# An attention block with two dense layers: the second layer's first pair split earlier, and its turns moved behind the next block product

## The reference

```python
def _moe_ref(x, w_in, w_out, s, b):              # first dense layer, d_ff 2048
    r = np.maximum(x @ w_in, 0.0)
    return (s * (r * r) + b) @ w_out

def _moe2_ref(x, w_in, w_out, g_ln):             # second dense layer, d_ff 1024
    h = x @ w_in
    e = np.exp(h - h.max(-1, keepdims=True))
    solu = h * (e / (e.sum(-1, keepdims=True) + 1e-09))
    mu, var = solu.mean(-1), ((solu - mu) ** 2).mean(-1)
    return ((solu - mu) / np.sqrt(var + 1e-06) * g_ln) @ w_out
```

## Time and profile before

| | |
|---|---|
| median of 3 runs | 860.84 us (860.62 to 861.01) |
| profiled execution | 860.25 us |
| its span in the trace | 858.0 us |
| PE busy | 843.0 us, 98% |
| DVE busy | 514.4 us, 60% |
| ACT busy | 339.7 us, 40% |
| POOL busy | 341.3 us, 40% |

### The profile page before, as it was taken

The page is one execution under the profiler, slowest core; times in us unless marked ns, Lnnn a source line. Parts: engine busy times, 40 slices in busy tenths (PEclk is TensorE's granted clock), DMA queues, the critical chain, the costliest instruction groups (busy, mean ns, idle before and its releaser), DMA issues.

```text
span 858.0 us, 13135 instructions
## 1 busy us (share of the span) xinstructions
PE 843.0 (98%) x4912; PEld 745.5 (87%) x4912; DVE 514.4 (60%) x1052; ACT 339.7 (40%) x607; POOL 341.3 (40%) x452
## 2 busy tenths in 40 slices
PE   8999999999999999999999999999999999999998
PEld 7899999999888888888888889999997878888886
DVE  7766657666547865433443344335767987777763
ACT  6665555556442223222322232224345433333322
POOL 5665656565659993000000000001548753334400
PEclk9999999999999999999999999999999999999999
DMA  8665666665403332000000000000101100000001
GB/s 147 147 144 130 152 140 140 145 132 126 118 14 98 111 99 74 1 0 1 1 1 0 1 1 1 1 1 1 50 26 50 36 26 25 26 24 13 25 25 49
DMA packets 86365, 49.35 MB, mean 58 GB/s; under 512 B 65056, under 2 KB 73248, under 8 KB 86304
## 3 DMA queue, kind: packets, MB, share of 16 engines
q1 hardware_dynamic: 83760, 47.94, 23.2%
q10 hardware_dynamic: 2544, 0.59, 0.4%
HBM read 27.28 MB, written 4.72 MB: 37 GB/s over the span
## 4 chain that ended last, share of the span: by engine, by line
PE 85%; DVE 10%; issue 3%; ACT 1%; POOL 1%; ACTq 0%; POOLq 0%; DVEq 0%
PE ps_h L1256 7%; PE ps_h L1257 7%; PE ps_h L1258 7%; PE ps_y L1271 7%; PE ps_y L1272 7%; PE ps_y L1273 7%; PE ps_v L650 7%; PE ps_s L565 4%; PE ps_r L1721 3%; PE ps_r L1720 3%; PE ps_r L1719 3%; PE ps_hid L1654 3%; PE ps_hid L1656 3%; PE ps_hid L1655 3%; DVE spent L967 3%
## 5 line engine op out<-in xcount | busy, mean ns | idle before, releaser
L1373 DVE TENSOR_TENSOR xT<-xT 128x512 f32<-128x512 f32 (+1 forms) x80 | 61.7, 772 | 125.6 <-ACT xT L1331 125.5
L1273 PE MATMUL ps_y<-g_hi,wout 128*128 128x512 f32 (+1 forms) x320 | 117.5, 367 | 0.0
L1272 PE MATMUL ps_y<-g_lo,wout 128*128 128x512 f32 (+1 forms) x320 | 117.5, 367 | 0.0
L1271 PE MATMUL ps_y<-g_hi,wout 128*128 128x512 f32 (+1 forms) x320 | 117.4, 367 | 0.0
L1557 POOL TENSOR_TENSOR win<-stage,win 128x512 fp32r<-128x512 f32 x2 | 2.6, 1296 | 281.8 <-ACT win L1788 281.8
L650 PE MATMUL ps_v<-v_raw,pT 128*128 128x65 f32 (+1 forms) x960 | 107.6, 254 | 1.2 <-DVE t_loc L1065 1.2
L650 PEld LDWEIGHTS ps_v<-v_raw,pT 128*128 128x128 f32 (+1 forms) x960 | 101.3, 173 | 6.9 <-issue 4.7
L967 DVE CUSTOM_DVE_ANT_0 spent<-ps_s,mask 128x576 f32<-128x576 f32 (+4 forms) x160 | 81.6, 540 | 42.4 <-PE ps_s L565 41.8
L1256 PE MATMUL ps_h<-x_hi,win 128*128 128x512 f32 (+1 forms) x280 | 103.0, 368 | 0.0
L1258 PE MATMUL ps_h<-x_hi,win 128*128 128x512 f32 (+1 forms) x280 | 102.8, 367 | 0.0
L1257 PE MATMUL ps_h<-x_lo,win 128*128 128x512 f32 (+1 forms) x280 | 102.8, 367 | 0.0
(11 more groups left out here) (211 smaller groups left out, 1805.1 us busy)
## 6 DMA issues: line engine op xcount, KB each, us to landing
stacked<-cut SPq DMA_DIRECT2D x56, 288.0 KB, 5.1
out<-res SPq DMA_DIRECT2D x18, 256.0 KB, 2.0
v_raw<-in_v SPq DMA_DIRECT2D x32, 128.0 KB, 3.2
stage<-in_moe_w_in SPq DMA_DIRECT2D x16, 256.0 KB, 2.7
stage<-in_moe_w_out SPq DMA_DIRECT2D x16, 256.0 KB, 2.6
k_raw<-in_k SPq DMA_DIRECT2D x28, 128.0 KB, 2.6
q_raw<-in_q SPq DMA_DIRECT2D x28, 128.0 KB, 3.6
stage<-in_moe_w_in SPq DMA_DIRECT2D x4, 512.0 KB, 3.5
```

Source lines behind the costliest of these rows:

```text
L1271: pe.matmul(out, wout[:, f, HI, w], g_hi[:, r, 0:n], start=(f == 0), stop=False)
L1272: pe.matmul(out, wout[:, f, HI, w], g_lo[:, r, 0:n], start=False, stop=False)
L1273: ins = pe.matmul(out, wout[:, f, LO, w], g_hi[:, r, 0:n], start=False, stop=(f == FT - 1))
L1373: dve.tensor_tensor(r, r, r, ALU.mult).then_inc(square_done, 1)
```

## The change

Three things are changed.

1. `round_y(0)` moves from the aside at f = 14 to the one at f = 12 on ScalarE, and `cut_lows(dve, 0)` from f = 14 to f = 13 on VectorE, ahead of low_crossed(1, BOTTOM). The rounding of pair 0 waits for output 9 of the last chunk in place of output 11; the cut of its low part now waits for output 10 and the cut of the sums' low part for output 11.
2. In the pairs p = 2 to 8 TensorE's `turn(a)` comes after `sums_product(p)`, and `turn(b)` after `shared_product(p)`.
3. In the same pairs VectorE does `join_first(p)` before both halves of `turned_low(a)`, and `join_shared(p)` before both halves of `turned_low(b)`.

No instruction of computation is added or removed.

```diff
     def y_is_free(eng, p):
         if p == 0:
-            freed.second_weights(eng, 11)
+            freed.second_weights(eng, 9)
...
         def cut_sums(p):
             y = y_of[p % 2]
+            if p == 0:
+                freed.second_weights(pool, 11)
             pool.wait_ge(s_hi_done, p + 1)
...
     def cut_lows(eng, p):
 
         y, a, b = y_of[p % 2], 2 * p, 2 * p + 1
+        if p == 0:
+            freed.second_weights(eng, 10)
         eng.wait_ge(y_hi_done, RAW * p + 1)
...
             upper_tile(p)
+            sums_product(p)
             turn(a)
-            sums_product(p)
             lower_products(p)
+            shared_product(p)
             turn(b)
-            shared_product(p)
             upper_ends(p)
...
             if f == 12:
                 high_crossed(1, TOP)
+                round_y(0)
             if f == 13:
                 round_sums(0)
                 high_crossed(1, BOTTOM)
-            if f == 14:
-                round_y(0)
...
             if f == 13:
+                cut_lows(dve, 0)
                 low_crossed(1, BOTTOM)
-            if f == 14:
-                cut_lows(dve, 0)
...
                 a, b = 2 * p - 2, 2 * p - 1
+                join_first(p)
                 turned_low(a, 0)
                 turned_low(a, 1)
-                join_first(p)
                 join_second(p)
+                join_shared(p)
                 turned_low(b, 0)
-                join_shared(p)
                 turned_low(b, 1)
```

## The result

| | before | after |
|---|---|---|
| median of 5 runs each | 861.01 us (860.62 to 861.76) | 856.79 us (856.63 to 857.42) |
| ratio | | 0.995, 95% interval 0.9936 to 0.9965 |
| profiled execution | 860.25 us | 856.63 us |
| its span | 858.0 us | 854.5 us |

The two traces differ by 3.5 us of span. In the later sessions 14 of 55 executions of the kernel before took 861.5 to 862.0 us, with a mean granted clock of 0.997 or 0.998, and the others 859.8 to 861.1 us, with 0.999 or 1.0, while none of the 77 executions of kernels with the earlier split showed less than 0.999; what ties the two together is not shown.

A forecast was written before the change was run, and what follows sets the result against it. TensorE, busy 98% of the span, was taken as the bound, so only its waits could be won: 1.6 + 1.36 = 2.9 us off 860.25 gives 857.3, plus 0.59 a median of 857.9 us; range 857.2 to 859.6.

The forecast's parts named there:

- Gap 1: TensorE's wait between output(4, 13) and upper_tile(0), 2.40 us with its slow first product; forecast to close wholly.
- What is queued behind: Load and pair 1's sums behind L1911 come 0.55 us later; exponentials(0) start at 658.15, only 0.7 earlier.
- The chain up to turn(2): VectorE from the exponentials on: join_second(1) and normalise(2) 1.55 us earlier, normalise(2) ending at 686.05.
- gap 2: TensorE's wait before turn(2) for a normalised tile, 1.08 us; 0.55 forecast to be left.
- the full 3.48: Both TensorE gaps closed, 2.40 + 1.08 us: the most the change can bring.
- Part 2: turn(a) behind sums_product(p): 1.36 us less TensorE work before turn(2); the six later pairs cost nothing.
- Rival D: Slower: turn(b) waits for tile a's low part behind join_first(p), one product each in seven pairs, 867.4 us; chance 0.04.
- From the span to the median: The median taken 0.59 us above the profiled execution, turning 857.3 into 857.9 us.
- B: Low cuts caught twice, GpSimd's scaling going ahead of L1911: gain 2.2 us, time 858.7; chance 0.22.
- C: The gap only changes place and only the turns' move pays: 1.08 to 1.36 us, time 859.5 to 859.8; chance 0.14.
- E: No effect: TensorE's waits come from something later than VectorE's low part, time stays 860.8 us; chance 0.02.

The follow-up runs named there:

- the split alone: Kernel before with only the earlier split and finer waits, TensorE's and VectorE's loops as before: 858.21 against 860.32 us, ratio 0.9972.
- the run with the sums first: Changed kernel with ScalarE rounding the sums at f = 12 and the rows at f = 13: 857.95 us against 860.60 for the kernel before.

## Why the prediction was wrong

The size was wrong, the direction and the places were right. Two terms of the sum were mis-sized. The first is the 1.6 us by which VectorE would be ahead at turn(2): it was 2.13. The second is the 0.59 us from the profiled execution to the median, which was 0.16 for the changed kernel. The paths of both follow.

**Gap 1** closed wholly, as forecast: pair 0 starts at 646.73 for 646.81 forecast. The split's placing was right; its gain in time alone is 2.1 us, which the run of the split shows.

**What is queued behind.** This step failed. I let the second cut be caught behind cut_sums; it was not, since VectorE's two cuts followed each other without a gap and GpSimd waited (2.68 for 2.40). I added 0.55 to the load and the sums; L1914 did end 0.34 later, at 646.09, but GpSimd went on only 0.19 later and made that up in its sums, whose first had met VectorE before and now did not (1.04 before, 0.73 after). That the first sum was longer because of VectorE is read off the overlap of the rows and was not tested. So exponentials(0) started at 657.56, not at 658.15.

**The chain up to turn(2).** "Only 0.7 earlier ... This is the step that limits the gain" was mis-sized. From the exponentials on I moved VectorE by 0.66 (for the 0.70 of the step before); spread_of(0) came 1.63 earlier (661.98 for 663.61): 1.3 of it from the exponentials themselves, and the rest because ScalarE's two exponentials now follow each other at once (VectorE's maxima are long done) and the multiplications and copies behind them take 3.20 (658.78 to 661.98) where they took 3.52 (660.09 to 663.61 in the trace of before). join_second(1) then came just as TensorE's product was ready, and moved by the full 2.42; the run with the weights behind the exponentials shows that this product is its limit. From there 0.3 were lost again, which I had not reckoned with: normalise(0) (L1973 at 665.62) now runs beside GpSimd's scaling (L1601, 664.88 to 666.25) and took 1.18, where it took 0.81 at 668.05 before, with the scaling over at 667.69. So VectorE was 2.13 earlier at turn(2); that the scaling is the cause is read off the overlap. The 0.55 us that I left of gap 2 were 0.06. That is 0.5 us of the error: the full 3.48, which I had as the upper bound, is what happened. That it came out so exactly is luck: the 2.13 and the 1.36 of sums_product(2) make 3.49, with nothing to spare. The two operations that meet, VectorE's and GpSimd's in the kernel after:

```profile
665.62 1.18 DVE L1973 TENSOR_SCALAR expo<-expo,small 128x1024 f32<-128x1024 f32 x1
```

```profile
664.88 1.37 POOL L1601 TENSOR_SCALAR stage<-stage,ln_gain 128x512 f32<-128x512 f32 x2
```

**Part 2** was right: 1.36 of work against a wait of 1.37 with the split alone, nothing in the later pairs, and the slack in both orders as computed there. Rival D's mechanism, a turn(b) that waits for tile a behind join_first, is real but needs one half of the change without the other: the run with TensorE's old order gives its price, 0.4 us a pair.

**From the span to the median.** I took the median of before, 860.84, 0.59 above its profiled execution, and kept this distance for the kernel after. There it was 0.16 (856.79 for 856.63), and the kernel before itself has medians of 860.3 to 861.0. With the right gain of 3.5 the forecast would have been 857.3, still 0.5 high by this step; the range allowed 0.15 for it. Half of the miss is in this, and by it alone the measured median lies outside the range, whose lower end already had the full 3.48.

Rivals B, C and E fell: L1914 ended at 646.1, join_second came with TensorE, and the waits went with their causes. Which of a VectorE and a GpSimd operation that hold each other up goes first was my main doubt. The traces show both orders: the square of block 13 (start 639.77) took 2.58 behind cut_sums (start 639.50) in the run with the sums first, and cut_sums gave way to two cuts in the changed kernel. The Trainium skill ("SBUF — State Buffer", "Who interferes with whom") says that of two such operations the one that issues second is blocked until the first has finished. In the changed kernel L1645 (641.74) had started before cut_sums (642.32), which agrees; that L1648 followed at 642.34, its duration unaffected, goes beyond what the rule tells, and only the trace showed it. It is no accident of one execution: cut_sums took 2.68 to 2.70 in every trace that has the two cuts ahead of it.

## What to carry to other kernels

When a critical engine is moved ahead by closing a gap, follow the next engine to the first place where it waits for the critical one again: there it moves by the whole shift, less what new collisions take behind it (2.42 at join_second(1), 2.13 at turn(2)), and a delay before it counts only beyond its slack. Moving a step behind independent work needed its partner on the other engine here: on top of the split alone the turns moved without the additions lose 3.8 us and the additions without the turns 2.6 to 2.9, and together they gain 1.2. And where the expected gain is near the scatter of the kernel before, give the median its own allowance.

## What the runs showed of the hardware

After a wait TensorE's first product of 512 columns is followed after 0.31 to 0.34 us in place of 0.23 (behind a turn, without a wait, after 0.31 to 0.32), so that a wait for which the profile lists 0.42, in the run with VectorE's old order, cost 0.69. And of two VectorE subtractions back to back the second was not held up by a GpSimd subtraction recorded 0.02 us before it (0.42, as in the kernel before); the GpSimd one was 0.28 longer.
